# Attention groups ahead of the first tile in plain fp32, four first-layer blocks collected beside them, another block order in that tile

## The reference

```python
# attention, for each chunk of 32 queries: 8 memory keys + 16 left + 32 own + 8 right keys
scores = scale * np.matmul(q_c, k_full.transpose(0, 1, 3, 2))
a = np.exp(scores - np.max(scores, axis=-1, keepdims=True))
a = a / (np.sum(a, axis=-1, keepdims=True) + 1e-09)
out[:, :, c_start:c_end] = np.matmul(a, v_full)
...
h = x @ w_in                                              # first network
g = np.maximum(h, 0.0) + alpha * np.minimum(h, 0.0)
x = g @ w_out
h = x @ w_in2                                             # second network
g = h * (1.0 / (1.0 + np.exp(-1.702 * h)))
out = g @ w_out2
```

## Time and profile before

| | us |
|---|---|
| median of 3 runs (1168.65 to 1170.19) | 1169.36 |
| the profiled execution | 1167.37 |
| its span in the trace | 1165.8 |
| PE busy | 1127.1 (97%) |
| DVE busy | 830.4 (71%) |
| ACT busy | 568.0 (49%) |
| POOL busy | 547.2 (47%) |

### The profile page before, as it was taken

How to read it: one execution, slowest core, us unless ns; L and a number is a source line. 1 busy time by engine, 2 the same in 40 slices (tenths; PEclk the granted TensorE clock), 3 DMA queues, 4 the chain that set the end, 5 groups by cost and what they waited for, 6 DMA issues and landing times.

```text
span 1165.8 us, 19123 instructions
## 1 busy us (share of the span) xinstructions
PE 1127.1 (97%) x6624; PEld 1037.5 (89%) x6624; DVE 830.4 (71%) x1209; ACT 568.0 (49%) x1230; POOL 547.2 (47%) x438
## 2 busy tenths in 40 slices
PE   4799999999999999999999999999999999999997
PEld 4788899999999999999999998888888888888886
DVE  7778577577577676676774535478879678897678
ACT  7656556465565565564564314534434434345330
POOL 6287266365465554562662722336433445243232
PEclk9799999999999999999999999999999999999999
DMA  5344144454354444442432507666687666667545
GB/s 195 115 161 140 67 135 163 153 172 163 130 162 143 150 162 150 153 163 76 144 133 83 197 1 257 190 194 196 187 268 242 218 192 195 195 203 254 161 158 167
DMA packets 84241, 192.00 MB, mean 165 GB/s; under 512 B 5824, under 2 KB 9920, under 8 KB 84160
## 3 DMA queue, kind: packets, MB, share of 16 engines
q1 hardware_dynamic: 67008, 153.12, 40.7%
q10 hardware_dynamic: 17152, 37.75, 9.3%
HBM read 148.91 MB, written 41.94 MB: 164 GB/s over the span
## 4 chain that ended last, share of the span: by engine, by line
PE 86%; DVE 5%; issue 3%; ACT 2%; DMA 2%; POOL 2%; ACTq 0%; SPq 0%; DVEq 0%
PE p_h L1080 7%; PE p_y L1096 7%; PE p_y L1098 7%; PE p_h L1082 7%; PE p_y L1097 7%; PE p_h L1081 7%; PE p_y L1106 6%; PE p_y L1108 6%; PE p_y L1107 6%; PE p_h L1108 3%; PE p_h L1106 3%; PE p_h L1107 3%; DMA w_raw<-weights 2%; PE p_score L1108 2%; PE p_turn L1108 2%
## 5 line engine op out<-in xcount | busy, mean ns | idle before, releaser
L471 POOL TENSOR_TENSOR gs_lo<-hidden,gs_hi 128x1024 fp32r<-128x1024 f32 x60 | 153.4, 2561 | 271.6 <-ACT gs_hi L673 271.6
L397 POOL TENSOR_TENSOR g_lo<-g_raw,g_hi 128x384 fp32r<-128x384 f32 x112 | 121.6, 1086 | 197.4 <-ACT g_hi L546 196.5
L1080 PE MATMUL p_h<-x_hi,w_hi 128*128 128x384 f32 x512 | 178.2, 348 | 3.9 <-DVE g_raw L802 2.6
L1096 PE MATMUL p_y<-g_hi,w_hi 128*128 128x384 f32 x512 | 176.6, 345 | 0.0
L1081 PE MATMUL p_h<-x_lo,w_hi 128*128 128x384 f32 x512 | 173.3, 338 | 0.0
L1082 PE MATMUL p_h<-x_hi,w_lo 128*128 128x384 f32 x512 | 173.2, 338 | 0.0
L1098 PE MATMUL p_y<-g_hi,w_lo 128*128 128x384 f32 x512 | 171.9, 336 | 0.0
L1097 PE MATMUL p_y<-g_lo,w_hi 128*128 128x384 f32 x512 | 171.8, 336 | 0.0
L546 ACT ACTIVATE g_hi<-g_raw 128x384 fp32r<-128x384 f32 x128 | 67.2, 525 | 189.0 <-DVE g_raw L802 188.7
L1106 PE MATMUL p_y<-gs_hi,down_ring 128*128 128x512 f32 x336 | 130.9, 390 | 2.1 <-DVE rest L924 2.1
L1108 PE MATMUL p_y<-gs_hi,down_ring 128*128 128x512 f32 x336 | 130.7, 389 | 0.0
(11 more groups left out here) (136 smaller groups left out, 2712.6 us busy)
## 6 DMA issues: line engine op xcount, KB each, us to landing
up_ring<-pairs SPq DMA_DIRECT2D x84, 512.0 KB, 3.7
down_ring<-pairs SPq DMA_DIRECT2D x84, 512.0 KB, 3.7
qkv_raw<-qkv SPq DMA_DIRECT2D x32, 576.0 KB, 3.8
qkv_other<-qkv SPq DMA_DIRECT2D x32, 576.0 KB, 3.8
pairs<-pair_split ACTq DMA_DIRECT2D x16, 1024.0 KB, 5.0
pairs<-pair_split ACTq DMA_DIRECT2D x16, 768.0 KB, 3.6
w_raw<-weights SPq DMA_DIRECT2D x16, 512.0 KB, 4.6
w_raw<-halves ACTq DMA_DIRECT2D x16, 512.0 KB, 5.8
```

Of the source, the lines that this page charges most:

```text
L397: pool.tensor_tensor(g_lo[:, f % GRING, :], g_raw[:, f % 2, :], g_hi[:, f % GRING, :], ALU.subtract).then_inc(g_lo_done, 1)
L471: pool.tensor_tensor(gs_lo[:, j], source, gs_hi[:, j], ALU.subtract).then_inc(gs_lo_pool, 1)
L1080: pe.matmul(o, w_hi[:, f, cols], x_hi[:, c, :], start=(c == 0), stop=False)
L1096: pe.matmul(o, w_hi[:, f, cols], g_hi[:, s, :], start=(f == 0), stop=False)
```

## The change

In the attention ahead of tile 0 the operands are no longer split. `score_first` multiplies the raw `q` and `k` in plain fp32 (4 matmuls instead of 8), `values_first` the raw `v` and the probabilities (4 instead of 12). All eight groups are loaded in one piece of SBUF, `raw_first`, which lies in the places of `w_hi` from block 7 on; only 64 partitions of `q` and `k` are loaded. The splits of `q`, `k`, `v` and of the transposed probabilities go, on ScalarE, VectorE and GpSimd. Each head's output goes from PSUM to `x_hi` and `x_lo` directly. The order of the loops becomes: TensorE `score(h)`, `turn(h-2)`, `values(h-2)`; VectorE `mask_scores(h)`, `normalise(h-1)`, `split_head_first(h-2)`; ScalarE a weight block, `split_head_first(h-2)`, `exponentials(h)`, `copy_turned_first(h-1)`. The rows of the scores have three sets of buffers.

At h = 4, 6 and 8 four up blocks (0 to 3) collect a chunk each, into `p_h` and two of the `p_y` banks. Six weight blocks are split beside the attention (`EARLY = 6`). In tile 0 the order is up 0 to 5, down 0 to 3, then up f and down f-2 as before; block i is split on GpSimd at step 2i-10, on ScalarE one step earlier, and loaded two steps earlier. The masking of a head's scores in tile 0 stands one step later on VectorE, and `leaky` of block f stands ahead of `split_g` of block f-1.

```diff
+AHEAD = 4
+FIRST_STEPS = [("up", _f) for _f in range(AHEAD + 2)] + [("down", _f) for _f in range(AHEAD)]
+for _f in range(AHEAD + 2, FB):
+    FIRST_STEPS += [("up", _f), ("down", _f - 2)]
+FIRST_STEPS += [("down", FB - 2), ("down", FB - 1)]
...
-EARLY, EARLY_AT = 3, 0
+EARLY = 6
+EARLY_AT = [0, 1, 2, 4, 5, 6]
+ROWS = 3
+def weights_at(i):
+    return 2 * i - 10
...
+        raw_first = at("raw_first", place["w_hi"] + (EARLY + 1) * 2 * MODEL * 4, [P, HEADS, QKV])
+        first_bank = [p_h[0], p_h[1], p_y[2], p_y[3]]
...
+            def load_first(h):
+                sp.dma_start(raw_first[0:D, h, 0:VO], qkv[h, 0:D, 0:VO]).then_inc(first_loaded[h], DMA)
+                sp.dma_start(raw_first[:, h, VO:QKV], qkv[h, :, VO:QKV]).then_inc(first_loaded[h], DMA)
...
+            load_first(0)
             load_weights(0)
+            load_first(1)
             load_weights(1)
             sp.dma_start(alpha_sb[:, :], alpha).then_inc(alpha_loaded, DMA)
+            load_first(2)
+            load_first(3)
+            load_weights(2)
+            load_first(4)
+            load_first(5)
+            load_weights(3)
+            load_first(6)
+            load_first(7)
+            load_weights(4)
             load_group(HEADS, 0)
             load_group(HEADS + 1, 1)
+            load_weights(5)
+            load_weights(6)
+            load_weights(7)
...
             for h in range(HEADS + 2):                      # ScalarE
+                for i in range(EARLY):
+                    if EARLY_AT[i] == h:
+                        split_weights(i)
+                if 0 <= h - 2:
+                    split_head_first(h - 2)
+                if h < HEADS:
+                    exponentials(h, rows_first[h % ROWS], rows_first[h % ROWS], h % ROWS)
+                if h == HEADS:
+                    act.wait_ge(qkv_loaded[0], DMA * (HEADS // 2 + 1))
+                    split_group(HEADS, 0, raw_of[0])
                 if 0 <= h - 1 < HEADS:
+                    copy_turned_first(h - 1)
...
             for h in range(HEADS + 2):                      # VectorE
                 if h < HEADS:
+                    mask_scores(h, 0, rows_first[h % ROWS], score_bank[h % 2], h % ROWS)
                 if 0 <= h - 1 < HEADS:
+                    normalise(h - 1, rows_first[(h - 1) % ROWS], (h - 1) % ROWS)
+                if h == HEADS + 1:
+                    split_q(HEADS, 0, raw_of[0])
+                if 0 <= h - 2:
+                    split_head_first(h - 2)
...
+            def score_first(h):
+                pe.wait_ge(first_loaded[h], 2 * DMA)
+                if h >= 2:
+                    pe.wait_ge(masked, h - 1)
+                for w in range(NW):
+                    last = pe.matmul(score_bank[h % 2][0:WQ, w * WK:(w + 1) * WK],
+                                     raw_first[0:D, h, QO + w * WQ:QO + (w + 1) * WQ],
+                                     raw_first[0:D, h, KO + w * WK:KO + (w + 1) * WK], start=True, stop=True)
+                last.then_inc(score_ready, 1)
+            def values_first(h):
+                pe.wait_ge(pt_hi_done, h + 1)
+                for w in range(NW):
+                    cols = slice(w * WQ, (w + 1) * WQ)
+                    last = pe.matmul(turn_bank[h % 2][0:D, cols], raw_first[:, h, VO + w * D:VO + (w + 1) * D],
+                                     turned_first[h % 2][:, cols], start=True, stop=True)
+                last.then_inc(head_ready, 1)
...
             for h in range(HEADS + 2):                      # TensorE
                 if h < HEADS:
+                    score_first(h)
                 if h >= 2:
+                    turn_first(h - 2)
+                    values_first(h - 2)
+                if h >= 4 and h % 2 == 0:
+                    for f in range(AHEAD):
+                        up(0, f, True, [(h - 4) // 2])
...
+                if first and f == 0:
+                    pe.wait_ge(g_done, H_FREE + AHEAD)      # in down_first
```

More of the change, by code:

```diff
@@ L452, in tile @@
                             split_kv(HEADS * t + HEADS + h, h, raw_of[h % 2])
-                    if first and kind == "up" and f + EARLY < FB:
-                        split_weights(f + EARLY)
+                    for i in range(EARLY, FB):
+                        if first and weights_at(i) == k:
+                            split_weights(i)
                     for i, u in enumerate(units):
@@ L507, in split_weights, with exponentials @@
                 act.activation(w_hi[:, i % FB, :], w_raw[:, i % 2, :], ACT.Copy).then_inc(w_hi_done, 1)
-            def exponentials(g, s=0, sets=1):
+            def exponentials(g, into, source, s=0):
                 act.wait_ge(shifted, g + 1)
-                if not (isinstance(g, int) and g < sets):
-                    act.wait_ge(turned, g - sets + 1)
+                if not (isinstance(g, int) and g < HEADS):
+                    act.wait_ge(turned, g)
                 for w in range(NW):
-                    last = act.activation(probs[s][:, w, :], scores[s][:, w, :], ACT.Exp,
+                    last = act.activation(into[:, w, :], source[:, w, :], ACT.Exp,
                                           bias=row_shift[:, s, w:w + 1],
@@ L618, in tile @@
                 g0 = HEADS * t + HEADS
-                if attention:
+                if attention and not first:
                     act.wait_ge(qkv_loaded[0], DMA * (HEADS // 2 * (t + 1) + 1))
@@ L640, in tile @@
                             split_group(g0 + h, h, raw_of[h % 2])
-                    if first and kind == "up" and f + EARLY < FB:
-                        split_weights(f + EARLY)
+                    for i in range(EARLY, FB):
+                        if first and weights_at(i) - 1 == k:
+                            split_weights(i)
                     for c in range(KC):
@@ L857, in tile @@
                 pending = None
-                if attention:
+                if attention and not first:
                     split_q(g0, 0, raw_of[0])
-                for k, (kind, f) in enumerate(STEPS):
+                for k, (kind, f) in enumerate(FIRST_STEPS if first else STEPS):
+                    if attention:
+                        for h in after(k, 2):
+                            normalise(g0 + h, probs)
+                    if kind == "up":
+                        leaky(FB * t + f, f, first)
                     if pending is not None and first:
@@ L864, in tile @@
                     if attention:
-                        for h in after(k, 2):
-                            normalise(g0 + h)
-                    if kind == "up":
-                        leaky(FB * t + f, f)
-                    if attention:
                         for h in after(k, TURN_LAG):
                             split_turned(g0 + h)
-                        for h in after(k, 0):
-                            mask_scores(g0 + h, (t + 1) % TPB)
+                        for h in after(k, 1 if first else 0):
+                            mask_scores(g0 + h, (t + 1) % TPB, scores, p_score)
                         for h in splits(k - 1):
@@ L1061, in values, with up @@
                     cols = slice(w * WQ, (w + 1) * WQ)
-                    o = turn_bank[s][0:D, cols]
-                    pe.matmul(o, vh, pt_hi[s][:, cols], start=True, stop=False)
-                    pe.matmul(o, vh, pt_lo[s][:, cols], start=False, stop=False)
-                    last = pe.matmul(o, vl, pt_hi[s][:, cols], start=False, stop=True)
+                    o = p_turn[0:D, cols]
+                    pe.matmul(o, vh, pt_hi[:, cols], start=True, stop=False)
+                    pe.matmul(o, vh, pt_lo[:, cols], start=False, stop=False)
+                    last = pe.matmul(o, vl, pt_hi[:, cols], start=False, stop=True)
                 last.then_inc(head_ready, 1)
-            def up(t, f, layer, chunks=range(KC)):
+            def up(t, f, first=False, chunks=range(KC)):
                 n = FB * t + f
-                pe.wait_ge(w_lo_done, FB * layer + f + 1)
-                if 0 in chunks:
+                pe.wait_ge(w_lo_done, f + 1)
+                if not (first and f < AHEAD):
                     pe.wait_ge(g_done, n + 1)
```

194 lines of the change are left out of this document (88 added, 106 removed).

## The result

| | before | changed |
|---|---|---|
| median, us | 1169.01 | 1175.52 |
| all runs, us | 1166.02 to 1170.20 (6) | 1173.23 to 1179.17 (6) |
| span of the profiled execution, us | 1165.8 | 1173.6 |
| first matmul, us | 8.04 | 4.40 |
| collected ahead of the rest of tile 0 | 2 blocks, 53.7 us | 4 blocks, 58.7 us |

The change makes the kernel slower: ratio 1.0064, 95% interval 1.0042 to 1.0086. 7.6 of the 7.8 us of span have been lost by the end of tile 0, as the first matmul of tile 1 shows.

A forecast was written before the change was run, and what follows sets the result against it. Losses lay before 144.10 us: TensorE waiting for VectorE, low clock, then the weight chain. Tile 0 ending at 136.0 instead of 144.1 gains 8.1: 1167.37 becomes 1159.3, plus 1.99 for the median 1161.3; range 1151.5 to 1169.0.

The forecast's parts named there:

- Start: Ahead of tile 0: splits before the first score go, TensorE starts at 4.2 us instead of 8.04, 3.8 us gained.
- VectorE, ScalarE, and the price of plain fp32: Attention, per head: VectorE 2.9 us, ScalarE 2.4 to 3.4; plain fp32 3.7 ns a column at the low level.
- The transpositions' row: Lower price for plain fp32, 1.6 ns a column low: scores 0.8 us, values 0.6, end 3 us earlier.
- The collected blocks and the clock: Attention: first chunk done at 26.6 us, high clock from about 27, four collected blocks done at 47.9 us.
- the high level from about 27: Attention: TensorE's clock granted in full from about 27 us, so the later chunks start at 32.6, 40.8 and 45.8.
- rival 3: Low clock through the whole attention: chunks end at 60.5 us, total 1173.9; chance 0.13 together with rival 4.
- rival 4: Attention: longer fp32 products replace the splits, 0.7 us more a head, total 1167.0; chance 0.13 together with rival 3.
- The rest of tile 0: After the attention: TensorE alone would end at 126.5 us, the later weight chain sets the end at 136.0.
- the cycle stays four steps of the list per two blocks: Tile 0's weight chain keeps 5.99 us a block: block 6 split near 49.8 us, block 15 at 103.7.
- Rival 2: Tile 0: weight chain slower behind group loads, 6.4 us a block, end at 141.3, total 1166.6; chance 0.15.
- The wait for `leaky` at up 4: Tile 0: up 4 needs `leaky` of blocks 0 to 2, done at 50.4 us; TensorE idles 2.6 us.
- Rival 1: Tile 0: weight chain does not bind with six blocks ahead; end 126.5 us, 17 us gained, 1152.3; chance 0.17.

The follow-up runs named there:

- filler: Changed kernel with five unused 128x128 matmuls per head from h = 3 on, between turn and values; 1177.32 us, ratio 1.0081.
- act_same_step: Changed kernel with ScalarE's weight-block split in tile 0 one step later, in the step of GpSimd's; 1167.87 us, ratio 0.9996.
- sync_ahead: Changed kernel with SyncE issuing each weight block in tile 0 one step earlier in its list; 1166.82 us, ratio 0.9994.
- fill_gaps: Changed kernel with the collected blocks put between turn and values, two at each head instead of four at every second; 1170.10 us, ratio 1.0015.
- fill_sync: Changed kernel with the edits of fill_gaps and sync_ahead together; 1160.50 us, ratio 0.9937.

## Why the prediction was wrong, point by point

I forecast 1161.3 us, 1151.5 to 1169.0, and faster with 0.8. It became 1175.5.

- **Start.** Right for the first score (4.40 against 4.2). Wrong behind it: the forecast has no term for the landing of groups 1 and 2, and its values of head 1 end at 18.2. TensorE stood 1.8 and 1.35 us for the two groups, which came at 8.20 and 11.56, and as the scores of head 2 stand ahead of the first transposition, those values ended at 21.4. I took smaller pieces to arrive sooner (they are 352 KB, not 360), and had no row for pieces of this form.
- **VectorE, ScalarE, and the price of plain fp32.** Right. On VectorE masking and maximum take 1.32 us, normalising 1.1, the head split 0.55; ScalarE's copies 0.48. Scores take 1.99 us low and 1.04 high against 1.9 and 1.0, values 1.47 against 1.4. The transpositions' row would have been too low by more than half. The Trainium skill's page FP8 and Floating Point Precision (TensorE Precision Notes) gives four passes for true FP32. The trace lies around that: the values, 3.83 ns a column, cost 3.4 times an fp32r product of the same 96 columns (0.107 us), the scores, 3.9 ns a column, 4.7 times the 0.83 of a 384-column one (0.32 us).
- **The collected blocks and the clock.** This is the first step that failed. The first chunk ran from 26.3 to 30.3 us, where I had 22.8 to 26.6: 3.7 us late, with the late groups. Then I took "the high level from about 27", though I had written, in rival 3, that every head keeps a gap. The clock rose at 30 and fell again at 37, 47 and 54, each time behind such gaps, and the last matmul ended at 58.7 instead of 47.9. That was rival 3, which I gave, with rival 4, 0.13. The clock is not all of the 10.8 us. The late groups are 3.7; the three later chunks took 3.8, 3.8 and 4.6 us, where at the high level (filler) they take 2.3, 2.2 and 3.1, so some 4.6 us. The rest is in handovers that I had at 0.3 us a head, such as 1.25 us before the last chunk for the last head's split, and in the 0.8 us of the next tile's first scores, which stand inside the last chunk. With the gaps filled the attention ended at 48.0. That this is my 47.9 is luck: the groups came as late there, and another order made up for it. In the order that I had priced, with the clock high and 35 matmuls more (filler), it was 55.1.
- **The rest of tile 0.** The second failed step: "the cycle stays four steps of the list per two blocks". I priced it at 5.99 us a block from the kernel before. It was 7.27: block 6 on ScalarE at 58.28, block 15 at 123.68, nine intervals. I moved ScalarE's split by one step and did not count the steps between SyncE's issue and ScalarE's wait, two before and one after, nor what stands in front of the issue (the group load, which waits for VectorE's split of `q`). Rival 2 named the group loads, but priced them at 6.4 us a block. act_same_step and sync_ahead show from both ends what it was worth: 7.6 and 8.7 us.
- **The sum, with the measured terms.** Block 6 came 8.5 us later than forecast (58.3 against 49.8), the nine intervals took 11.5 us more (65.4 against 53.9), the way from there to the end 4.3 less (28.0 against 32.3): 15.7 us, which is 151.7 against 136.0.
- **The wait for `leaky` at up 4** was 1.1 us instead of 2.6 (2.1 in fill_gaps, filler, act_same_step, sync_ahead and fill_sync). No run tests the moved masks and the moved `leaky` by themselves.
- **Rival 1** (the chain does not bind) is right about ScalarE in the mended versions, whose waits for weights fall to 0.8 us in fill_sync, but not about the end: 136.3 there, 132.6 with block 6 ahead, and not 126.5. The attention ended 2.9 us later than in that sum, and TensorE still waits for heads taken (3.3 us), turned rows and scores (1.7 each), which the sum left out.
- Both failed steps work at once and in different stretches. I had given them as rivals with a chance each; the measured time is above all of them because they add.

## What to carry to other kernels

When a consumer's step is moved earlier in its list, count the steps between the issue of its transfer and its wait, and look at what the issuing queue waits for in front of it: here a third free buffer gave nothing, since the issue stood behind another load. When TensorE gets short gaps in a stretch, put independent work into the gaps rather than behind them; here the same matmuls in another order took 11 us off a stretch of 59, by using the gaps and by keeping the clock up. When a forecast rests on the clock being high, price the stretch at the low level first. And try the cheap edit on the kernel before as well: here one moved loop there (1161.4) was worth as much as the large change with both faults mended (1160.5).

## What the runs showed of the hardware

- With gaps of 0.58 to 1.5 us a head in the attention the granted clock fell (0.67 and 0.76 at 36 to 42 us), while with 35 short matmuls in them it stayed at 1.00. It is not the same each time: in act_same_step the same attention kept 1.00 over 36 to 42 us behind the same gaps, and fell to 0.59 and 0.50 over 42 to 48.
- In the first 30 us of the changed kernel the granted clock reads 1.00 while matmuls of 384 columns stand 0.32 us apart; there the distance between two starts is to be believed, not the column.
- Transfers of 224 and 128 KB (64 partitions of 3.5 KB, and 128 of 1 KB) landed 5.2 and 5.7 us after their issue in the first 30 us (medians), two for each group. The single ones of 576 KB took 6.5 us, and brought the second and third group sooner.
- A plain fp32 matmul stands in the trace as two records, a transposition of fp32 as one. Per column a plain fp32 matmul costs 4.7 times (low level, 3.9 against 0.83 ns) and 4.5 times (high, 2.03 against 0.45) what a 384-column fp32r matmul does, and 3.4 times what an fp32r product of its own 96 columns does (low, 0.37 against 0.107 us).
